# VectorE takes the second product out of PSUM in ScalarE's place, in a fused recurrence, MLP and expert kernel

## The reference

```
new_re = ar * S_re - ai * S_im ;  new_im = ar * S_im + ai * S_re
S_re = new_re + k v^T ;  y[t] = q[t] S_re
x  = y reshaped to (3072, 384)
h  = x @ w_in ;  g = h * tanh(softplus(h)) ;  x2 = g @ w_out
logits = x2 @ w_gate + modality_bias[modality_id] ;  e = argmax(logits)
out[token] = softmax(logits)[e] * (relu(x2 @ w1[e]) @ w2[e])
```

## Time and profile before

| | us |
|---|---|
| median of 3 runs | 1104.81 |
| lowest, highest run | 1103.52, 1107.12 |
| the profiled execution | 1103.16 |
| its span in the profile | 1101.4 |
| PE busy | 980.2 (89%) |
| DVE busy | 712.3 (65%) |
| ACT busy | 625.5 (57%) |
| PE's share of the chain that ended last | 84% |

### The profile page before, as it was taken

One profiled execution on the slowest core, in us unless ns is written; L12 is line 12 of the kernel. 1 busy time (PEld: TensorE's weight loads), 2 busy tenths in 40 slices (PEclk: granted clock), 3 DMA queues, 4 the chain that ended last, 5 costly groups with the idle time before them and its releaser, 6 DMA issues.

```text
span 1101.4 us, 19052 instructions
## 1 busy us (share of the span) xinstructions
PE 980.2 (89%) x6516; PEld 946.6 (86%) x6517; DVE 712.3 (65%) x1288; ACT 625.5 (57%) x1185; POOL 80.6 (7%) x138
## 2 busy tenths in 40 slices
PE   2557989999999999999999999995279999879996
PEld 0446889899999999999999999994269999879996
DVE  4363479898888897888897876775533333463332
ACT  5353668687677787677777765561034444444442
POOL 1000000000000000000000000000012222322222
PEclk9985889999999999999999999997669999999999
DMA  6521011112112122122121110000151111331110
GB/s 179 152 51 36 16 23 37 37 37 58 37 37 58 37 51 57 33 43 58 38 58 37 22 44 8 1 22 24 65 194 36 43 36 43 137 134 43 41 38 29
DMA packets 146164, 58.66 MB, mean 53 GB/s; under 512 B 131257, under 2 KB 140487, under 8 KB 146096
## 3 DMA queue, kind: packets, MB, share of 16 engines
q1 hardware_dynamic: 139280, 42.63, 16.0%
q0 software_dynamic: 3616, 10.43, 3.0%
q10 hardware_dynamic: 3200, 4.72, 1.2%
HBM read 48.21 MB, written 10.03 MB: 53 GB/s over the span
## 4 chain that ended last, share of the span: by engine, by line
PE 84%; DVE 6%; issue 3%; ACT 2%; DMA 2%; SPq 1%; ACTq 0%; POOL 0%; POOLq 0%; DVEq 0%
PE bank L1342 19%; PE bank L1323 18%; PE bank L1491 13%; PE bank L1502 10%; PE bank L1295 4%; PE bank L1263 3%; PE bank L1297 3%; PE bank L1271 3%; PE bank L1281 3%; PE bank L1249 1%; PE bank L1243 1%; PE bank L1358 1%; PE bank L1312 1%; PE bank L1474 1%; SPq L414 1%
## 5 line engine op out<-in xcount | busy, mean ns | idle before, releaser
L1491 PE MATMUL bank<-xg_t,w_sb 128*128 128x128 f32 x1296 | 157.4, 283 | 18.3 <-ACT he L784 16.9
L1491 PEld LDWEIGHTS bank<-xg_t,w_sb 128*128 128x128 f32 x1296 | 155.8, 199 | 19.5 <-ACT he L784 17.8
L1323 PE MATMUL bank<-x_hi,w_in_hi 128*128 128x384 f32 x384 | 142.3, 370 | 5.6 <-DVE w_in_lo L927 5.6
L1342 PE MATMUL bank<-w_out_hi,g_hi 128*128 128x392 f32 x384 | 141.1, 367 | 0.0
L1323 PE MATMUL bank<-x_lo,w_in_hi 128*128 128x384 f32 x384 | 131.6, 343 | 0.0
L1323 PE MATMUL bank<-x_hi,w_in_lo 128*128 128x384 f32 x384 | 131.5, 343 | 0.0
L1342 PE MATMUL bank<-w_out_hi,g_lo 128*128 128x392 f32 x384 | 130.6, 340 | 0.0
L1342 PE MATMUL bank<-w_out_lo,g_hi 128*128 128x392 f32 x384 | 130.5, 340 | 0.0
L627 ACT ACTIVATE hid<-bank 128x384 f32<-128x384 f32 x128 | 62.4, 488 | 90.7 <-PE bank L1323 89.8
L784 ACT ACTIVATE he<-bank 128x128 f32<-128x128 f32 x216 | 59.5, 277 | 65.9 <-PE bank L1491 59.5
L1212 DVE TENSOR_SCALAR he_m<-he 128x256 int32<-128x256 int32 x108 | 31.8, 294 | 78.8 <-ACT he L784 78.8
(11 more groups left out here) (208 smaller groups left out, 2106.8 us busy)
## 6 DMA issues: line engine op xcount, KB each, us to landing
w_sb<-in_moe_w_dram SPq DMA_DIRECT2D x8, 1536.0 KB, 7.2
ab<-in_a_re_dram SPq DMA_DIRECT2D x24, 192.0 KB, 2.9
ab<-in_a_im_dram SPq DMA_DIRECT2D x24, 192.0 KB, 3.1
qk_raw<-in_q_dram SPq DMA_DIRECT2D x24, 192.0 KB, 3.1
qk_raw<-in_k_dram SPq DMA_DIRECT2D x24, 192.0 KB, 3.3
v_in<-in_v_dram SPq DMA_DIRECT2D x24, 192.0 KB, 2.7
x_rows<-x_sb ACTq DMA_DIRECT2D x8, 576.0 KB, 3.0
w_in_sb<-in_moe_w_in_dram SPq DMA_DIRECT2D x4, 768.0 KB, 8.7
```

The costliest lines, as they stand in the source:

```text
L1323: last = mm(bank_h[f % 2][:, 0:TT], w[:, kk, f * P:(f + 1) * P], x[:, m % 2, kk], start=(kk == 0 and i == 0), stop=(kk == KD - 1 and i == 2))
L1342: last = mm(bank_x2[t][:, 0:DE], g[:, u % RING, f % QF, t * P:(t + 1) * P], w[:, f], start=(f == 0 and i == 0), stop=(f == FT - 1 and i == 2))
L1491: last = mm(bank_h[f % 2][:, 0:P], w1_sb[par][:, kk, f * P:(f + 1) * P], xg_t[:, kk], start=(kk == 0), stop=(kk == KD - 1))
```

## The change

The six copies of a block's x2 and logits move from ScalarE to VectorE, at the same gap number, 18, of VectorE's own list. ScalarE keeps the DMA that stores the rows and issues it in gap 22. For the last block VectorE copies after its last `times` and before it loads the flag `slow`; ScalarE issues the store where it copied before.

```
-            def take_x2(m):
-                act.wait_ge(second_done, NQ * (m + 1))
-                wait(act, x2_out, 16 * m)
-                for t in range(G3):
-                    act.activation(logits[:, m * G3 + t], bank_x2[t][:, DM:DE], ACT.Copy).then_inc(x2_copied, 1)
-                    act.activation(x2_sb[:, t], bank_x2[t][:, 0:DM], ACT.Copy).then_inc(x2_copied, 1)
+            def put_x2(m):
                 act.wait_ge(x2_copied, 2 * G3 * (m + 1))
                 act.dma_start(x2_rows[0:N].rearrange("(m g p) d -> m p g d", p=P, g=G3)[m], x2_sb[:]).then_inc(x2_out, 16)
...
-                    if g == X2_AT and m:
-                        take_x2(m - 1)
+                    if g == X2_AT + 4 and m:
+                        put_x2(m - 1)
                     if g % 2 == 0:
                         take(m, g // 2)
...
             slow = act.value_load(slow_i[0:1, 0:1], min_val=0, max_val=MAX_FLAGS)
-            take_x2(NT - 1)
+            put_x2(NT - 1)
...
+            def take_x2(m):
+                dve.wait_ge(second_done, NQ * (m + 1))
+                wait(dve, x2_out, 16 * m)
+                for t in range(G3):
+                    dve.tensor_copy(logits[:, m * G3 + t], bank_x2[t][:, DM:DE]).then_inc(x2_copied, 1)
+                    dve.tensor_copy(x2_sb[:, t], bank_x2[t][:, 0:DM]).then_inc(x2_copied, 1)
...
+                    if g == X2_AT and m:
+                        take_x2(m - 1)
                     if x < NCH and p == FRAC_AT:
...
             times(NT * NQ - 1)
+            take_x2(NT - 1)
             dve.wait_ge(slow_known, 1)
             slow = dve.value_load(slow_i[0:1, 0:1], min_val=0, max_val=MAX_FLAGS)
```

## The result

The changed kernel took 1117.96 us, the median of four runs (1115.54, 1115.68, 1120.24 and 1120.48). The kernel before, in four runs, had a median of 1104.16 (1097.51 to 1107.12). The ratio is 1.0134, with a 95% interval of 1.0078 to 1.0189: slower by 1.3%. (The ratios and intervals in this document compare runs of the same batch; they are not quotients of the two medians, which would be 1.0125 here. Before's own median was between 1099.56 and 1104.77 us in the later batches.) The forecast was 1116.9, from 1113 to 1122. The profiled execution took 1115.54 us with a span of 1113.8, against 1103.16 and 1101.4 before: 12.4 us more in the span.

What follows compares the result with a forecast made beforehand. PE, busy without a pause from 252 to 728 us, was taken to bound the kernel. Waits of 11.3 us plus 0.25 and 0.5 after the slots made 12.1, added to the median 1104.81: 1116.9 us, range 1113 to 1122.

Steps and rivals of the forecast that it cites:

- 1.59 five times, 1.17 and 2.22: Slots 1 to 5, 6 and 7: microseconds PE loses waiting for VectorE's copies to free bank 5; 11.3 us together.
- the handover: In the slots: PE starts 0.06 us after the end of the VectorE instruction it waited for.
- The start behind the pair: Gap 18 on VectorE: the copies start 1.74 us after the pair L866 starts, estimated as 1.82 less 0.08.
- the spacing of the banks: VectorE's copies in the slots: each next bank follows some 0.54 us later, from 0.07 and 0.56 less 0.09 overlap.
- ScalarE's idle 0.39 us: Gap 13: ScalarE idles for PE's transposes L1263, so VectorE's lateness follows PE's and the loss recurs in each slot.
- lost once only: Slots: if VectorE's own backlog sets its pace, PE loses 1.59 us once and 0.63 in slot 7; 1107.8 us, chance 0.05.
- Copies end to end: VectorE's copies start only at the earlier one's end, holding PE 2.02 us in five slots; 1120.4 us, chance 0.10.
- the price, 3.1 us a time: Clock rival: loss per fall, from the first 36 L1491 taking 7.11 us after long idleness against 4.02.
- the rival: Slots: PE's waits bring the granted clock down to half, 1.2 GHz, seven times; 1138.6 us, chance 0.02.
- +0.75: After the slots: 0.25 us for VectorE's copies plus 0.5 us for the load of the flag, added to the forecast.
- The 0.25 for slower copies: After the slots: VectorE's six last copies end at 757.12 where ScalarE's ended at 756.87, +0.25 us.
- The 0.5 for the flag's register: After the slots: the flag's load into a register now follows the copies; 0 to 1.11 us, taken as 0.5.

Runs made afterwards that it cites:

- e10: The changed kernel with VectorE's copies between the two scaled operations of gap 17 in slots 1 to 6, slot 7 as in the change; 1111.0 us, ratio 1.0073.
- e1: The changed kernel with VectorE's x2 copies two gaps earlier, behind the attention's work of gap 16; 1100.61 us, ratio 0.9984.
- e2: The changed kernel with VectorE's x2 copies one gap earlier, at the head of gap 17; 1105.8 us, ratio 1.0017.
- e5: The changed kernel with only the last block's copies back on ScalarE; 1115.34 us in one run.
- e12: The changed kernel run once more with no edit; 1115.23 us in one run.
- e6: The kernel before with only the last block's six copies moved to VectorE, ahead of the load of the flag; 1106.08 us in one run.

## Why the prediction came out right

**The slots.** Right in mechanism and nearly in size. Predicted 1.59 five times, 1.17 and 2.22, together 11.34; measured 1.64 or so, 1.23 and 2.32, together 11.75. The term that was off is the handover: 0.06 us was read from PE's one wait, on another kind of operation; behind these copies it is 0.15 in slot 1, and again in e10. The start behind the pair (1.74 us) and the spacing of the banks (0.54) held to 0.01. That the loss recurs in each slot, which was argued from ScalarE's idle 0.39 us, held to 0.02 us, so "lost once only" is out. e1 and e2 show the same from the other side: two gaps or one earlier, and nothing is lost in slots 1 to 6.

**Copies end to end.** Out: the starts are 0.07 and 0.47 apart behind durations of 0.15 and 0.54. The prediction took one sentence on the pipe from the Trainium skill's section "The DRAIN you can't avoid" of the page "VectorE: DVE Perf Modes". That section also says that a next operation which isn't held starts earlier, and this the trace bears out; weighing the first sentence by itself made a rival of something the page doesn't claim of such copies.

**The clock.** Here the prediction failed, in two steps. I argued from a single wait of 2.06 us at clock 1.00 that waits of this size bring no fall. One wait was no evidence, and not for being rare: that wait is in all thirteen profiles and the clock never fell behind it, so more of the same would have misled as well (the last section shows what sets it apart). In the three profiles with all seven waits (after, e5, e12) ten falls stand behind twenty-one waits. The second step was the price, 3.1 us a time, taken from a stretch after long idleness; here a fall costs 1.56. So the rival came true in part, at 3.1 us in the first profile and 6.2 in the second, where 21.7 had been set against it.

**After the slots.** The sum had +0.75 and the stretch became 2.31 us shorter. The 0.25 for slower copies is right (0.25 and 0.19). The 0.5 for the flag's register is wrong as a term of the sum, not as a duration: the load takes 0.55 us, and the trace does show it, but it runs beside the copies. With it e6 would have been 0.75 longer than before, and it is 0.19 longer, which the copies alone explain. What dominates is a cost that I did not see standing in the row of before: 3.3 us between the last copy and L1100, marked only as "issue", were for 2.6 us (3.26 less 0.70 from the jump on) a load of code, and the longer program of the change happened to do without it. The step that failed is to take the gap of before as a fixed amount and only add to it.

**The rest.** From the routing on, after has 1.6 us more (342.8 against 341.2), and slot 0's x2 came 1.8 us earlier. Kernels whose program is the same there reach from 340.3 to 342.9 in the table. The length goes with the clock: in that stretch it was granted at its lower level for 63.4 to 66.4 us in the seven profiles that take 342.1 to 342.9, after among them, and for 55.6 to 61.7 us in the six that take 340.2 to 341.6, before among them. Why there is more of it in the one than in the other stays open, and so does the start.

So the span's 12.4 us are: waits 11.75, two clock falls 3.12, the last stretch 0.07, after the slots -2.31, routing and experts 1.58, start -1.81. The forecast of 12.1 is close in its sum because what it left out cancels: the clock's 3.12 against the lost code load and the 0.75 that it had added there, and the routing and experts against the start. It was right for its main reason, and lucky beside it.

None of these kernels can be told to be faster than before. The best form of the change is e1: with the copies two gaps earlier it is level with before (0.9984), while the change as it stands is at 1.0134.

## What to carry to other kernels

Ask of a moved step when its new engine comes to it and when the buffer is wanted, not how full that engine is: the same copies cost 11.8 us, 6.5 (e10) or nothing (e1) in the slots by where they stand within two gaps of VectorE's list. A price for a wait on PE should have a second figure beside it, for the slow products that may follow. And a gap marked "issue" behind a jump isn't fixed: any edit that changes the length of an engine's program can add or drop a load of code there, so compare it apart from the edit's own work.

## What the runs showed of the hardware

The granted clock fell behind some of PE's waits and not behind others of the same length at the same place of the same program. In after, e5 and e12 it fell behind 8 of the 15 waits of 1.43 to 1.45 us, behind none of the three of 1.03, and behind 2 of the three of 2.14 or 2.15; with e2 and e10 the last are 3 of 5. Behind the six waits of 0.57 us or less in e10 it never fell.

What picks among them can be read from the records of the granted clock. In each of the thirteen profiles all its changes, those of the start and of the experts too, lie on one even grid, to 0.001 us. Against a program's first instruction the grid lies differently each time. Of the 15 waits of 1.43 to 1.45 us, the eight with a fall are those behind which the next point of the grid came 0.13 to 0.80 us after the wait's end; the fall began at that point. Of the seven without, five had a point inside the wait, and behind two it came 0.87 and 1.82 us after the end. Of the five waits of 2.14 or 2.15 us, two with a fall had no point inside and the third had one only 0.07 us after its start; the two without had a point well inside. The old wait of 2.06 us had a point inside in all thirteen profiles. e5 and e12 lie against the grid alike (within 0.02 us at slot 0's x2) and fell in the same four slots; the first profile of the change lies 0.4 us off and fell in slots 1 and 2. No run moved the grid on purpose, so this is read from the traces and not tested. The Trainium skill, page "TensorE: Matmul & The Clock Gate", section "What's actually happening", says that the watch on TensorE's activity runs freely and does not start anew with a kernel; with this the trace agrees.

A code load of 8 KB behind VectorE's jump over a part that is never run (the `If` at L1092) held up its next instruction by 2.4 to 2.6 us, and 42 more instructions ahead of the jump, copies in the slots or memsets, took it out of the way.

VectorE's sequencer goes ahead of its engine: it took 0.55 us to load a flag into a register while the engine made its copies, and that cost nothing.
